# A masked-attention front end rebuilt as 24 unrolled units on one Trainium2 core

## The reference, cut to what matters

```python
batch, n_heads, seq, head_dim = 4, 8, 576, 64
scores = q @ k.T / 8
rel = pos[:, None] - pos[None, :]
plain   = (rel >= 0) & (rel < 32)                        # heads 0 to 3
dilated = (rel >= 0) & (rel < 128) & (rel % 4 == 0)      # heads 4 to 7
attn = exp(where(mask, scores, -1e9) - max) ; attn /= attn.sum(-1) + 1e-9
x = (attn @ v) as 2304 tokens x 512
# then: each token goes to one of 8 experts (512 -> 1024 relu -> 512), scaled by its gate,
# then one dense layer pair (512 -> 2048 softplus -> 512) for all tokens
```

## Time and profile before

| what | value |
|---|---|
| median of 3 runs | 814.34 us (813.33 to 814.98) |
| the profiled execution's own time | 813.36 us |
| its span, first to last instruction | 811.6 us |
| PE busy | 762.9 us, 94% |
| DVE busy | 446.1 us, 55% |
| ACT busy | 398.4 us, 49% |
| POOL busy | 235.2 us, 29% |

### The profile page before, as it was taken

One profiled execution on the slowest core, in us unless ns is written; L12 is line 12 of the kernel. 1 busy time (PEld: TensorE's weight loads), 2 busy tenths in 40 slices (PEclk: granted clock), 3 DMA queues, 4 the chain that ended last, 5 costly groups with the idle time before them and its releaser, 6 DMA issues.

```text
span 811.6 us, 14035 instructions
## 1 busy us (share of the span) xinstructions
PE 762.9 (94%) x4658; PEld 688.8 (85%) x4659; DVE 446.1 (55%) x910; ACT 398.4 (49%) x1014; POOL 235.2 (29%) x218
## 2 busy tenths in 40 slices
PE   5999996399999999999899999999999999999996
PEld 3667665289999999999899999999999989999995
DVE  8985986864665577767663343343334343334332
ACT  3995894034553566655563453353344344335332
POOL 6220220544666559777830010010010001001001
PEclk9999998589999999999999999999999999999999
DMA  9677202354654666775400010000000000001000
GB/s 247 182 186 271 115 0 117 90 166 152 215 176 136 200 206 192 232 217 181 132 26 1 1 39 0 0 39 0 0 26 13 0 0 39 0 0 39 0 0 39
DMA packets 27258, 74.55 MB, mean 92 GB/s; under 512 B 4112, under 2 KB 12320, under 8 KB 26720
## 3 DMA queue, kind: packets, MB, share of 16 engines
q1 hardware_dynamic: 20624, 53.52, 21.1%
q0 software_dynamic: 5744, 16.02, 6.7%
q10 hardware_dynamic: 864, 4.72, 1.5%
HBM read 64.79 MB, written 9.45 MB: 91 GB/s over the span
## 4 chain that ended last, share of the span: by engine, by line
PE 88%; DVE 7%; issue 2%; ACT 2%; POOL 0%; DVEq 0%; ACTq 0%
PE bank L620 13%; PE bank L622 13%; PE bank L621 13%; PE bank L644 8%; PE bank L646 8%; PE bank L642 8%; PE bank L633 4%; PE bank L635 4%; PE bank L634 4%; PE bank L499 4%; PE bank L523 2%; PE bank L536 2%; PE bank L509 2%; PE bank L606 1%; ACT probs L761 1%
## 5 line engine op out<-in xcount | busy, mean ns | idle before, releaser
L1237 DVE SCALAR_TENSOR_TENSOR g_sb<-bank,soft 128x384 f32<-128x384 f32 x96 | 53.6, 558 | 235.0 <-ACT soft L908 235.0
L904 ACT ACTIVATE soft<-bank 128x384 f32<-128x384 f32 x96 | 47.3, 492 | 208.7 <-PE bank L622 208.7
L471 POOL DMA_INDIRECT out<-y_sb,out_rows_i x18 | 17.5, 971 | 374.9 <-ACT y_sb L915 371.2
L1099 DVE TENSOR_TENSOR w_lo<-raw,w_hi 128x1024 fp32r<-128x1024 f32 x68 | 93.6, 1378 | 50.5 <-ACT w_hi L824 50.4
L620 PE MATMUL bank<-x_parts,w_hi 128*128 (+1 forms) x352 | 111.8, 318 | 3.7 <-DVE w_lo L1099 2.5
L622 PE MATMUL bank<-x_parts,w_lo 128*128 (+1 forms) x352 | 110.9, 315 | 0.0
L621 PE MATMUL bank<-x_parts,w_hi 128*128 (+1 forms) x352 | 110.8, 315 | 0.0
L824 ACT ACTIVATE w_hi<-raw 128x1024 fp32r<-128x1024 f32 x68 | 71.8, 1058 | 50.4 <-PE bank L635 49.6
L406 POOL TENSOR_SCALAR xs_sb<-landing,row_scale 128x256 f32<-128x256 f32 x48 | 64.3, 1348 | 65.8 <-PE bank L606 65.7
L633 PE MATMUL bank<-h_hi,w_hi 128*128 128x384 f32 (+3 forms) x256 | 80.7, 315 | 1.9 <-DVE h_lo L1119 1.9
L761 ACT ACTIVATE probs<-bank,neg_max 96x128 f32<-96x128 f32 x192 | 67.4, 366 | 22.5 <-DVE neg_max L950 22.5
(11 more groups left out here) (201 smaller groups left out, 1776.8 us busy)
## 6 DMA issues: line engine op xcount, KB each, us to landing
raw<-we SPq DMA_DIRECT2D x64, 512.0 KB, 3.5
x_tokens<-x_sb ACTq DMA_DIRECT2D x6, 768.0 KB, 5.1
v_sb<-vw SPq DMA_DIRECT2D x4, 1024.0 KB, 13.6
raw_m<-wm POOLq DMA_DIRECT2D x8, 512.0 KB, 5.2
raw<-wm SPq DMA_DIRECT2D x8, 512.0 KB, 3.6
q_sb<-qT SPq DMA_DIRECT2D x4, 768.0 KB, 9.1
k_sb<-kT SPq DMA_DIRECT2D x8, 384.0 KB, 11.4
v_sb<-vw SPq DMA_DIRECT2D x4, 512.0 KB, 4.7
```

Of the source, the lines that this page charges most:

```text
L1099: nc.vector.tensor_tensor(w_lo[:, r, :], raw[:, r, :], w_hi[:, r, :].bitcast(F32), ALU.subtract).then_inc(w_lo_done, 1)
```

## The change

- **Scores on row halves.** K is kept unpadded, one load in place of two. Each head's scores are one matmul of 64 rows and 128 columns. The two heads of a pair stand on rows 0 to 63 and 64 to 127 and go to different banks, so a half is now the even heads or the odd heads of all four pairs; one mask matmul writes two heads with the plain and two with the dilated mask.
- **Who does what.** GpSimd multiplies both halves by the inverse sums. VectorE forms the inverses of a unit's two halves in one pair of instructions and multiplies no more. It copies the even heads' transposed probabilities, ScalarE the odd heads'.
- **Order.** The two turns are unrolled to 24 units. Thirteen token tiles are put into units 8 to 11, 14 to 18 and 20 to 23, one in each; five follow the last unit. In a unit with a tile TensorE does the tile first and the scores of unit u+2 last, and VectorE takes the maxima of unit u+2 last. In the other units the scores come first, and the maxima right behind the inverses.
- **Start.** VectorE zeroes the masks in place of K's padding, makes several constants and spreads two index tables that GpSimd made whole before. TensorE's first scores wait for the first mask only.

The diff, cut to its core, in the order SyncE, GpSimd, TensorE (scores and order), ScalarE's order, VectorE's order:

```diff
-                for par in range(2):
-                    r = slice(D * par, D * (par + 1))
-                    sp.dma_start(k_sb[m][r, :, par, lo:hi], kT[b][r, :, lo:hi]).then_inc(loaded, 16)
+                sp.dma_start(k_sb[m][:, :, lo:hi], kT[b][:, :, lo:hi]).then_inc(loaded, 16)
...
+            for n in range(2 * ALL_UNITS):
+                c = n % BANKS
+                pool.wait_ge(inv_ready, n // 2 + 1)
+                nc.gpsimd.tensor_tensor(probs[:, c, :, :], probs[:, c, :, :],
+                                        inv_sum[:, c, :].unsqueeze(2).to_broadcast([QT, HEADS, KEYS]), ALU.mult
+                                        ).then_inc(normed[n % 2], 1)
...
+            def scores(u):
...
+                for par in range(2):
+                    if u > 1:
+                        pe.wait_ge(exps_done, 2 * (u - 2) + par + 1)
+                    if g is not None:
+                        pe.wait_ge(x_copied_dve if par else x_copied_act, g + 1)
+                    nc.tensor.matmul(banks[par][0:QT, :], identb[:, :], mask, start=True, stop=False,
+                                     skip_group_check=True)
+                for c in range(HEADS):
+                    for par in range(2):
+                        r = slice(D * par, D * (par + 1))
+                        last = nc.tensor.matmul(banks[par][0:QT, KEYS * c:KEYS * (c + 1)],
+                                                q_sb[m][r, c, q0:q0 + QT], k_sb[m][r, c, k0:k0 + KEYS],
+                                                start=False, stop=(c == HEADS - 1), skip_group_check=True)
...
+            for u in range(ALL_UNITS):
+                g = TILE_OF_UNIT.get(u)
+                if g is not None:
...
+                    pe.wait_ge(exps_done, 2 * u + 2)
+                    token_tile(g)
+                elif u + 2 < ALL_UNITS:
+                    scores(u + 2)
+                if u:
+                    values(u - 1)
+                for par in range(2):
+                    transposes(2 * u + par)
+                if g is not None and u + 2 < ALL_UNITS:
+                    scores(u + 2)
+            values(ALL_UNITS - 1)
+            for g in LATE_TILES:
+                pe.wait_ge(x_copied_act, g - 1)
+                pe.wait_ge(x_copied_dve, g - 1)
+                token_tile(g)
...
+            for u in range(ALL_UNITS):
+                g = TILE_OF_UNIT.get(u)
+                if u + 1 < ALL_UNITS:
+                    exps(2 * u + 2)
+                if g is not None:
+                    x_copy(g)
+                if u + 1 < ALL_UNITS:
+                    exps(2 * u + 3)
+                if u:
+                    dilated_tokens(u - 1)
+                odd_copies(u)
+                if g is not None and g % TILES_STORED == TILES_STORED - 1:
+                    x_store(g)
...
+            for n in range(BANKS):
+                maxima(n)
+            for u in range(ALL_UNITS):
+                g = TILE_OF_UNIT.get(u)
+                more = u + 2 < ALL_UNITS
+                inverses(u)
+                if g is not None:
+                    x_copy(g)
+                elif more:
+                    for par in range(2):
+                        maxima(2 * (u + 2) + par)
+                if u:
+                    plain_tokens(u - 1)
+                copies(2 * u)
+                if g is not None and more:
+                    for par in range(2):
+                        maxima(2 * (u + 2) + par)
```

More of the change, by code:

```diff
@@ L67 @@
 TILES_TURN = 2 * S // P
+ALL_UNITS = B * UNITS
 TILES_STORED = 3
@@ L226, in build @@
         sizes_ready = sem("sizes_ready")
+        x_stored = [sem(f"x_stored{n}") for n in range(3)]
         raw_loaded = [sem(f"raw_loaded{r}") for r in range(RING)]
@@ L481, in _ @@
         def _(pe):
[L483 to L510, removed]
-                last.then_inc(transposes_done, 1)
[L513 to L526, removed]
@@ new lines, in transposes, with values @@
+            def transposes(n):
+                u, par = n // 2, n % 2
+                pe.wait_ge(normed[par], u + 1)
+                if u:
+                    pe.wait_ge(pt_copied[par], u)
+                for c in range(HEADS):
+                    last = nc.tensor.transpose(pt_ps[par][:, QT * c:QT * (c + 1)], probs[:, n % BANKS, c, :],
+                                               ident[0:QT, 0:QT])
+                last.then_inc(transposes_done, 1)
+            def values(u):
+                b, i = u // UNITS, u % UNITS
+                for par in range(2):
+                    pe.wait_ge(pt_copied[par], u + 1)
+                if i == 0:
+                    pe.wait_ge(first_values_loaded[b % 2], 16 * (b // 2 + 1))
+                for c in range(HEADS):
+                    half, place = c // 2, 2 * QT * (u % 2) + QT * (c % 2)
+                    if u and c % 2 == 0:
+                        pe.wait_ge(out_copied_to_x[half], u)
+                    for par in range(2):
+                        last = nc.tensor.matmul(o_ps[half][D * par:D * (par + 1), place:place + QT],
+                                                v_sb[b % 2][:, i, 2 * c + par, :], probsT[:, par, c, :],
+                                                start=True, stop=True, skip_group_check=True)
+                    if c % 2:
+                        last.then_inc(values_done, 1)
@@ L535, in token_tile @@
+            def token_tile(g):
+                pair = pair_of_tile(g)
+                for half in range(2):
+                    pe.wait_ge(out_copied_to_x[half], units_behind(g))
+                t = g % TILES_TURN
                 for k in range(KC):
-                    last = nc.tensor.matmul(x_ps[t % 2][k // 2][:, TW * (k % 2):TW * (k % 2 + 1)],
+                    last = nc.tensor.matmul(x_ps[pair][k // 2][:, TW * (k % 2):TW * (k % 2 + 1)],
                                             xT_sb[:, k, P * t:P * (t + 1)], id_wg[:, k, :], start=True, stop=True,
@@ new lines, in _ @@
+            for par in range(2):
+                exps(par)
+            for u in range(ALL_UNITS):
[11 more added lines that the diff above has]
+                    x_store(g)
@@ L941, in _, with maxima @@
             dve.sem_inc(g_done, G_CREDIT)
-            def maxima(turn, n):
+            dve.wait_ge(indices_ready, 1)
+            nc.vector.tensor_copy(column_no[:, :, :], column[:, :].unsqueeze(2).to_broadcast([P, P, NT]))
+            nc.vector.tensor_copy(block_row[:, :, :], blocks[:, :].unsqueeze(1).to_broadcast([P, NT, BLOCKS])
+                                  ).then_inc(indices_spread, 1)
+            def maxima(n):
                 c = n % BANKS
-                dve.wait_ge(scores_done, turn * HALVES + (n + 1))
+                dve.wait_ge(scores_done, n + 1)
@@ L1008, in _ @@
+            plain_tokens(ALL_UNITS - 1)
+            for g in LATE_TILES:
+                x_copy(g)
             steps = [0]
```

301 lines of the change are left out of this document (128 added, 173 removed).

## The result

| | before | after |
|---|---|---|
| median | 814.39 us (813.33 to 814.98, 4 runs) | 824.61 us (822.94 to 825.49, 4 runs) |
| ratio | | 1.0124 [1.0105, 1.0144] |
| span of the profiled execution | 811.6 | 823.3 |
| the routing's first step (L1022, now L1038) | 134.56 | 145.10 |
| behind that step | 677.0 | 678.2 |

Slower by 10.2 us where 4.8 were forecast (814.3 to 819), inside the range and on the side that was given 0.65. The routing's step moved by 10.5 where 4.8 were worked out; another 1.2 came behind it.

What follows compares the result with a forecast made beforehand. TensorE was taken to bound the kernel (busy 94%) and pace the attention; start, plain units, tile units and tail summed to L1022 at 139.4 against 134.56, +4.8, hence a median of 819 us, range 811 to 828.

Steps and rivals of the forecast that it cites:

- the side that was given 0.65: Whole kernel: the predicted sign, slower, with chance 0.65, against faster 0.18 and same 0.17.
- Part 1: Attention scores: a pair's two heads run side by side, 0.87 us a unit; a block of scores takes 1.58.
- The middle case: Scores: loads of Q, an estimated 80 ns each, go one by one and cost 1.28 us a unit.
- Part 2: GpSimd multiplies both halves, 2.08 us a pair, blocking VectorE's small L950 throughout; plain units take 4.0.
- rival 1: Plain units: L950 slips in between GpSimd's two multiplies; units average 3.65, total +1.5, median 815.8 us; chance 0.22.
- ScalarE's 3.73: Attention units: ScalarE's work per unit, from 18.28 busy of 20 us, taken as the pace if L950 slips in.
- The 2.60 of the earlier trace: VectorE's L1099 at 221.17, 1.22 undisturbed, waited through GpSimd instructions; taken as evidence for plain units of 4.0.
- Part 3: Units with a tile: one chain through four engines takes 6.15 us, where a unit and its tile cost 5.16 before.
- Part 4: The start: first exponentials from 10.6 us, inverses(0) at 13.9, inverses(1) at 17.7; second pipeline filling gone.
- the other cases: Whole kernel: anything else, such as TensorE's clock falling in the tile units' gaps of 1.5; chance 0.05.
- its 139.4: Routing's first step, L1022: forecast start in us, against 134.56 before, +4.8.

Runs made afterwards that it cites:

- the reversed loop: Against the changed kernel, scores go through all four even heads, then all four odd heads, so neighbours stand on the same array rows; 847.66 us, one run.
- the version with VectorE's multiply: Changed kernel with separate semaphore for V's rest, next inverses ahead of maxima in tile units, and VectorE multiplying the even half in all units; 806.63 us, ratio 0.9923.
- V's rest apart: Against the changed kernel, the transfer of the rest of V gets its own semaphore, so scores wait for Q and K alone; 822.89 us, ratio 1.0038.
- TensorE kept busy: Against the changed kernel, eighteen small unused bf16 matmuls in each tile unit fill TensorE's waits for GpSimd; 820.85 us, ratio 1.0029.
- the inverses first: Against the changed kernel, in tile units VectorE forms the inverses of unit u+1 ahead of the maxima of u+2; 807.88 us, ratio 0.986.
- the even half on VectorE: Against the changed kernel, VectorE multiplies the even half again and GpSimd keeps the odd half; 811.65 us, ratio 0.9959.

## Why the prediction was right in direction and short in size

**Part 1** held. Two row halves side by side gave 0.057 from record to record where 0.054 was taken, and the reversed loop showed the alternative, 0.091. The block took 1.67 for 1.58. The middle case, loads that go one by one, did not come. By the Trainium skill ("TensorE: Matmul & The Clock Gate", LDWEIGHTS) a load takes its columns at 1.2 GHz, an estimated 80 ns for 96; sixteen loads a block did not space the records wider than 57 ns.

**Part 2** held in the 2.08 of the pair and failed in its choice between 4.0 and rival 1. L966 slips in between the two multiplies, and of three plain units two last 3.97 and one 3.17 (the six from 25.16 to 47.37 average 3.70, and rival 1 said 3.65). This step overstated the time by 3.2 in ten plain units. ScalarE's 3.73, worked out from a busy share, was no lower bound: the version with VectorE's multiply has plain units of 3.47 in a row. The Trainium skill ("SBUF — State Buffer", Who interferes with whom) has the lock held for a whole instruction; the trace agrees on that (a negation that began at 26.66 took 1.04, to the end of the second multiply), and on its coming free between two of GpSimd's. It agrees only roughly the other way round: GpSimd's multiply, begun with 0.64 of VectorE's to go, took 0.50 longer. The 2.60 of the earlier trace rows, which decided the choice, was one row of another operation, shape and type against a rule and a mechanism; what held it up there was not tried.

**Part 3** held and is the main cause: 6.21 for 6.15, link by link. Cutting the chain at the maxima brought tile units from 6.21 to 4.84 and took some 11.8 from the routing's step, beside the clock's share; shortening its GpSimd link by 0.50 took 0.49 from each unit. So the overlap of tiles with the attention was not the loss. Its order was: of the 5.16 that a unit and its tile cost before, 4.84 is possible.

**Part 4** failed in one link. The exponentials began at 9.92 (10.6 forecast), inverses(0) at 13.56 (13.9), but inverses(1) at 20.87 instead of 17.7. The scores of unit 2 wait for the semaphore of Q, K and the rest of V, and the working took K's and Q's bytes as all that matters. In the kernel before the same wait was 0.4 long, in front of a later start; an earlier start met it in full, 3.80, and the block behind it ran at 1.2 GHz. Apart, it gave 4.1 back.

**The clock** was the largest failed term of the sum, put at nothing. The forecast took the granted clock of 1.00 of a stretch where TensorE had almost no idle time for units that give it 1.7 us of waits each, and left the fall to the other cases with 0.05. Four tile units with records at 1.2 GHz brought +1.36, +1.5, +1.5 and +0.6: 5.0. Two profiles of the changed kernel and one with V's rest apart have three or four such units of eleven each, the two with TensorE kept busy none, those with the inverses first or the even half on VectorE none. That filling or shortening the waits removes the falls from the tile units is shown by this. Why some units of a kind fall and others do not is not shown, and the reversed loop shows that the clock can be low without any wait.

Together: +3.2 at the start, +5.0 by the clock, -3.2 in plain units and +0.7 of small differences (unit 17's gap 0.2, the chain's 0.06 in eleven units) make the 5.7 by which the routing's step missed its 139.4. With plain units sized right the forecast would have been 9 short at the step; that it lies inside its range is in part luck, since one error hid another. Behind the step 1.2 more was lost, against the assumption that nothing changes there, and 1.5 in the second profile. In the first it lies in the dense layers: from their first record to the end 410.9 instead of 409.8, with record durations of 1.2 GHz for 5.9 us near their start where the kernel before has them for 3.2. In the second 1.7 lies ahead of them, where TensorE waits 3.96 instead of 1.91 for VectorE's h_lo (L1135); why was not tried. The profiled execution lies 11.7 above its counterpart, the medians 10.2.

## What to carry to other kernels

When work is overlapped, write out each loop of waits through all engines and ask which instruction stands in it only by its place in an engine's order: moving two small instructions ahead of two maxima was worth more than the change's whole loss. When a start is made earlier, read every semaphore that the next steps wait for and what else it counts, since a wait that was covered is not any more. A clock read in one stretch need not hold in another that loads TensorE differently: here it fell when gaps came.

## What the runs showed of the hardware that was not expected

- TensorE fell to 1.2 GHz in units of 6.2 us in which it was busy 8.65 of 11 us and its longest wait was 1.21.
- In the reversed loop it kept the durations of 1.2 GHz past the block at 61.89 (2.99) without idle time, and was at full pace at 72.45 (1.63). The profile's granted clock says 1.00 throughout, from 20 to 75. The durations of records of a known kind (the mask pair, 0.59 or 1.06) tell the clock better than that column in the first stretch of a trace.
- GpSimd's multiply of 1.04 took 1.54 beside VectorE's multiply of 0.69 and slowed VectorE's not at all.
- The second multiply of a GpSimd pair lets a small VectorE instruction in before it: the negation of 0.17 ended 0.03 behind the first multiply.
- Column for column, 64-row fp32 matmuls of 128 columns start 0.091 apart on one row half, 0.71 ns a column, where the 256-column ones over all rows had 0.85.
